# One expert's second-layer weights read and rounded in halves, and scatters moved behind GpSimd's mask in a three-layer kernel

## The reference, cut to what matters

```python
# 4 batches, 8 heads, 768 steps, 48 per head
for t in range(S):
    state = alpha[:, :, t, :, None] * state + einsum('bhd,bhe->bhde', k[:, :, t], v[:, :, t])
    y[:, :, t] = einsum('bhd,bhde->bhe', q[:, :, t], state)
x = y.transpose(0, 2, 1, 3).reshape(3072, 384)
# experts: each token goes to the expert of its largest logit
logits = (x / norm(x)) @ (emb / norm(emb)).T / tau
idx, gate = argmax(logits), softmax(logits) at idx
out[tokens of e] = gate * (maximum(x @ w1[e], 0) @ w2[e])     # w1 384x1024, w2 1024x384
# feed-forward, 384 -> 2048 -> 384
h = out @ w_in
y = where(h > 0, h, exp(minimum(h, 0)) - 1) @ w_out
```

## Time and profile before

| | us |
|---|---|
| median of 3 runs (lowest, highest) | 894.9 (894.73, 895.32) |
| the profiled execution | 891.97 |
| its span on the core | 890.3 |
| TensorE busy in it | 867.2 |
| VectorE, ScalarE, GpSimd busy | 433.6, 326.7, 284.2 |

### The profile page before, as it was taken

The page is one execution under the profiler, slowest core; times in us unless marked ns, Lnnn a source line. Parts: engine busy times, 40 slices in busy tenths (PEclk is TensorE's granted clock), DMA queues, the critical chain, the costliest instruction groups (busy, mean ns, idle before and its releaser), DMA issues. The chain is left out here.

```text
span 890.3 us, 16092 instructions
## 1 busy us (share of the span) xinstructions
PE 867.2 (97%) x5725; PEld 774.7 (87%) x5725; DVE 433.6 (49%) x810; ACT 326.7 (37%) x698; POOL 284.2 (32%) x276
## 2 busy tenths in 40 slices
PE   8999999899999999999999999999999999999996
PEld 6888887689989998998988989899989999899985
DVE  7889898752232232232226445445445445445442
ACT  4576667732223222222222323233223323233322
POOL 3235655464755574285517102002002002002001
PEclk9999999999999999999999999999999999999999
DMA  9976774778778878757517002002002002000001
GB/s 151 164 145 127 175 155 104 271 237 283 232 245 274 297 206 270 244 153 212 161 54 234 16 1 72 0 1 72 1 1 72 1 1 72 1 0 31 7 1 36
DMA packets 140575, 106.35 MB, mean 119 GB/s; under 512 B 103338, under 2 KB 129058, under 8 KB 140498
## 3 DMA queue, kind: packets, MB, share of 16 engines
q0 software_dynamic: 24896, 62.95, 22.3%
q1 hardware_dynamic: 115602, 42.37, 21.3%
HBM read 87.94 MB, written 17.35 MB: 118 GB/s over the span
## 5 line engine op out<-in xcount | busy, mean ns | idle before, releaser
L1463 POOL DMA_INDIRECT out<-of,idi x24 | 26.8, 1115 | 364.0 <-ACT of L1569 300.8
L1276 PE MATMUL bank<-WX,hdTh 128*128 (+1 forms) x496 | 128.7, 340 | 0.5 <-PEq L448 0.5
L1505 PE MATMUL bank<-xT_h,wi_h 128*128 128x512 f32 x288 | 114.1, 396 | 0.0
L1505 PE MATMUL bank<-xT_l,wi_h 128*128 128x512 f32 x288 | 113.6, 395 | 0.0
L1505 PE MATMUL bank<-xT_h,wi_l 128*128 128x512 f32 x288 | 113.3, 393 | 0.0
L1575 ACT ACTIVATE ee<-bank 128x512 f32<-128x512 f32 x96 | 57.5, 599 | 146.7 <-PE bank L1505 144.6
L1597 DVE TENSOR_SCALAR em<-ee 128x512 f32<-128x512 f32 x96 | 44.2, 460 | 136.3 <-ACT ee L1575 134.8
L1260 PE MATMUL bank<-WX,xdTh 128*128 (+1 forms) x372 | 99.7, 403 | 3.6 <-ACT xdTh L1304 2.0
L1578 ACT ACTIVATE g_h<-gg 128x512 fp32r<-128x512 f32 x96 | 60.7, 632 | 114.9 <-DVE gg L1602 113.2
L1195 POOL TENSOR_TENSOR WX<-raw_w,WX 128x3072 fp32r<-128x3072 f32 x14 | 95.6, 6830 | 15.9 <-DMA WX<-moe_w 12.6
L1606 DVE TENSOR_TENSOR g_l<-gg,g_h 128x512 fp32r<-128x512 f32 x96 | 68.5, 713 | 60.3 <-ACT g_h L1578 59.4
(11 more groups left out here) (215 smaller groups left out, 1442.0 us busy)
## 6 DMA issues: line engine op xcount, KB each, us to landing
WX<-moe_w POOLq DMA_DIRECT2D x13, 1536.0 KB, 9.8
raw_w<-moe_w POOLq DMA_DIRECT2D x13, 1536.0 KB, 7.7
xd<-sorted_x SPq DMA_DIRECT2D x31, 193.0 KB, 5.3
sorted_y<-yd SPq DMA_DIRECT2D x31, 192.5 KB, 4.1
xg<-sorted_y SPq DMA_DIRECT2D x6, 770.0 KB, 4.6
nat_a<-alpha SPq DMA_DIRECT2D x32, 144.0 KB, 4.2
nat_k<-k SPq DMA_DIRECT2D x32, 144.0 KB, 3.5
nat_q<-q SPq DMA_DIRECT2D x32, 144.0 KB, 4.5
```

Source lines behind the costliest of these rows:

```text
L1276: last = pe.matmul(y_out(t)[:, 0:DM], hdT[a][:, k * P:(k + 1) * P], WX[:, bass.ds(off + (b * WE + KD * F + k * DM), DM)], start=(k == 0 an ...
L1505: last = pe.matmul(bank[4 + i % 2][:, :], a[:, k, w], b[:, k, :], start=(k == 0 and m == 0), stop=(k == KD - 1 and m == 2))
```

## The change

It has four parts.

1. The first expert's w2 is loaded in two DMAs of 4 of its 8 blocks each (`raw_half`), with a semaphore each, instead of in one.
2. ACT rounds it in two steps of 128x1536, `Wc0` and `Wc1`. `Re0` of tile 0 and `Gq` stand between them; before, they stood behind the whole. DVE's `W3`, `W4` wait for `Wc0`, and `W5`, `W6` for `Wc1`.
3. In POOL's rounds 8 and 12, one scatter instead of three stands ahead of the mask `M1`, and the other two stand behind `Zm`. In round 14 one instead of two stands ahead of the mask, and five instead of four behind `Gm`. These three rounds are all in which the built order differs.
4. In round 14 DVE's `LA` moves from ahead of the state steps to behind `Qh1`.

```diff
@@ steps_ve
             if n == PAIRS - 2:
-                out_ = [("M0", n)] + [(x, n + 1) for x in ("G", "Kh0", "Kh1")] + [("LA", n - 1)] + sums
-                out_ += [(x, n + 1) for x in ("R", "F", "Qh0", "Qh1")] + [("Y8", PARTIAL - 1)]
+                out_ = [("M0", n)] + [(x, n + 1) for x in ("G", "Kh0", "Kh1")] + sums
+                out_ += [(x, n + 1) for x in ("R", "F", "Qh0", "Qh1")] + [("LA", n - 1), ("Y8", PARTIAL - 1)]
...
@@ steps_po
-                    out_[0:0] = [("SC", b * C + j) for j in range(2)]
-                    out_ += [("SC", b * C + j) for j in range(2, C)] + [(f"X{i}", b) for i in range(X_STEPS)]
+                    out_[0:0] = [("SC", b * C)]
+                    out_ += [("SC", b * C + j) for j in range(1, C)] + [(f"X{i}", b) for i in range(X_STEPS)]
...
                 elif b < PARTIAL - 1 and r == 4:
                     i = place_of(out_, "M1")
-                    out_[i:i] = [("SC", b * C + j) for j in range(HC, C)]
+                    out_[i:i] = [("SC", b * C + HC)]
+                    i = place_of(out_, "Zm") + 1
+                    out_[i:i] = [("SC", b * C + j) for j in range(HC + 1, C)]
...
@@ ve_a
                     if x:
-                        acA.wait(ve, "Wc", 0)
+                        acA.wait(ve, "Wc0" if i < 5 else "Wc1", n)
...
@@ ac_a
                 if kind == "Wc":
-                    ac.wait_ge(s_raw0[1], 16)
-                    return ac.activation(parts_of(0)[0][:, W12[1]], raw[1][:, :], ACT.Copy)
+                    ac.wait_ge(s_raw0[1 + i], 16)
+                    cols = slice(i * KF * DM // 2, (i + 1) * KF * DM // 2)
+                    return ac.activation(parts_of(0)[0][:, W12[1]][:, cols], raw[1][:, cols], ACT.Copy)
...
-                    if name == "Wc":
+                    if name == "Wc0":
                         d(("Re0", 0))
...
+        def raw_half(eng, e, i, done):
+
+            ks = slice(i * KF // 2, (i + 1) * KF // 2)
+            return eng.dma_start(in_three(raw[1][:, :], 1)[:, ks, :], from_dram_x(e, 1)[:, ks, :]).then_inc(done, 16)
...
@@ sp_d
-            raw_load(sp, e, 1, s_raw0)
+            for i in range(2):
+                raw_half(sp, e, i, s_raw0[1 + i])
```

More of the change, by code:

```diff
@@ L256, in build @@
         s_scat = [sem(f"s_scat{b}") for b in range(BATCHES)]
-        s_raw0 = [sem(f"s_raw0_{x}") for x in "12"]
+        s_raw0 = [sem(f"s_raw0_{x}") for x in ("1", "2a", "2b")]
         s_raw1 = [sem("s_raw1_1")]
@@ L302, in build @@
         ROUTE_PE = [({}, {"YN1": ("CT",)})] * (BATCHES - 1) + [({"YN1": ("CT",)},)]
-        ROUTE_AC = [({}, {}, {}, {"Kt1": ("Gq",)})] * (BATCHES - 2) + [({}, {}, {"Kt1": ("Gq",)}), ({"Ln0": ("SL0",), "Yn1": ("SL1",), "Ln1": ("Wc", "Gq")},)]
+        ROUTE_AC = [({}, {}, {}, {"Kt1": ("Gq",)})] * (BATCHES - 2) + [({}, {}, {"Kt1": ("Gq",)}), ({"Ln0": ("SL0",), "Yn1": ("SL1",), "Ln1": ("Wc0", "Gq", "Wc1")},)]
         ROUTE_PO = [({"Zm": ("ID",)},)] * BATCHES
```

## The result

The changed kernel takes 899.0 us (898.2 to 899.8, 6 runs) against 895.2 us (894.7 to 897.3, 6 runs) of the kernel before: a ratio of 1.0041, 95% interval 1.0031 to 1.0051. It is slower by 0.3 to 0.5%; 892.0 with a range of 890.9 to 893.9 had been forecast. Its profiled execution took 899.78 us.

What follows compares the result with a forecast made beforehand. TensorE, busy 97% of the span, was taken as the bound, so only its waits could be won. Terms 1.14 + 0 + 0 + 1.74 = 2.88 us took the median from 894.9 to 892.0, range 890.9 to 893.9.

Steps and rivals of the forecast that it cites:

- Rounds 8 and 12, 1.14 us: With the mask in time, KV to the next KT becomes 3.60 us as in round 10: 0.61 + 0.53 won.
- Rounds 9 and 13, 0 us for the moved scatters: The moved scatters land before ACT's Yn0 would be delayed (up to 102.56 in round 9), so they cost 0.
- The two rivals built on it: Moved scatters of rounds 8 and 12 held by VectorE's scan: one held, 893.6 us (0.12); both held, 896.1 us (0.06).
- the slower one: Both moved scatters held in each of two rounds, 4.1 us lost against 2.88 won: 896.1 us, chance 0.06.
- Round 14, 0 us, bounds 0 and 0.6: The third mask wait, some 0.6 us, goes, but the wait at 168.72 grows by as much: 0 won.
- the wall that is w1's load: ACT's rounding of w1 starts at 160.25 only when its load has landed, so round 14's saving stops there.
- the hold by the scan from round 8: The scatter at 92.73 took 2.20 us against 0.96 during VectorE's long scan; a moved one might be held too.
- w2 in halves, 1.74 us: The first half lands at about 169.9, so tile 0's relu wait goes: 1.74 us won, bounds 1.3 and 1.74.
- Tile 2: Rival: the relu's gain is given back at tile 2's weight load if the last scatters come no earlier: 893.5 us (0.10).
- A slower result: Whole kernel above 896.7 us, expected only in the far end of the slow case: chance 0.04.

Runs made afterwards that it cites:

- no14: Changed kernel without its part in round 14 (halves of w2, one scatter each of rounds 8 and 12 moved): 889.9 us, ratio 0.9972 to the kernel before.
- la_only: Kernel before with only LA moved behind Qh1 in round 14: 895.4 us, ratio 1.0000.
- sc14_spaced: Kernel before with one scatter of round 14 moved behind the mask, and the third behind it waiting for VectorE's scan: 892.55 us, ratio 0.9997.
- r14_w1late: Kernel before with round 14's scatter and LA moved, and w1's load issued only when Ys1 of round 14 is done: 903.1 us (one run).

## Why the prediction was wrong, by its own steps

- **Rounds 8 and 12, 1.14 us.** The mask was in time in every kernel that moves it. On a chip like the profile's the term is right: rounds 8 and 12 are 0.61 and 0.49 us shorter in no14. On the chips that timed the change it is worth nothing (1.0002): with the two scatters behind the mask `KV`'s hand-over is late (state copies 2.1 to 2.4 us behind `KV` in round 8 and 1.6 to 2.3 in round 12, against 0.91 in both in la_only). Only one profile was at hand, and it lay 2.9 us below the median of the runs. The prediction shifted its sum by that difference; it should have asked whether the waits it removes exist in the slower executions. They mostly don't in that form: in la_only `Yi1` of round 8 waits for no mask, and the loss stands between `KT` and `KV`, 7.72 us instead of 5.73:

```profile
94.56 0.94 PE L713 MATMUL bank<-mix,yts 128*128 128x128 f32 x6 [0.44 <-ACT asb L956]
...
97.05 0.79 PE L667 MATMUL bank<-vn,ktsb 128*64 128x48 f32 x20
```

- **Rounds 9 and 13, 0 us for the moved scatters.** The landing was in time; ScalarE's `Yn0` waits for no DMA there. The two rivals built on it, the slower one among them, didn't occur. But the step priced a scatter by when it lands, and not by what it does while it is issued.
- **Round 14, 0 us, bounds 0 and 0.6.** This is the step that failed. The mask wait went, 0.67 us (8.93 instead of 9.60). The five scatters behind it then cost 5.4 us in round 15 and turned the sum. The lower bound of 0 rested on the wall that is w1's load, so on the belief that nothing but the load could come later. The prediction knew of the hold by the scan from round 8 (the 2.20 us of the earlier trace rows) and took it for a danger to the landing; in round 14 the same hold was the pause that kept the row harmless. With a pause put back the term comes out as forecast: in sc14_spaced round 14 is 0.6 us shorter, and the time is that of the kernel before (0.9997).
- **w2 in halves, 1.74 us.** Mechanism and size are right. Alone it gives 1.4 us (0.5 to 2.1 by the interval), in the trace 1.77 up to the transposes of `hd`, with the half landing 2.05 us ahead of the whole where 2.1 was estimated. In the whole change it gave nothing, since the relu wait would have gone anyway with the lateness of round 15.
- **Tile 2.** Nothing was given back there: from tile 0's transposes to the end it is 713.4 us instead of 714.8.
- **The chances.** A slower result had 0.04, from a single mechanism at the landing. The case that came was in no rival. The sum of the parts that were right (no14, 2.6 us won on a chip that runs like the profile, forecast 2.88) shows that the arithmetic held there. What was missing was a term in round 14, and on the slower chips one in rounds 8 and 12 too.

Open: why TensorE's results are released late while GpSimd issues scatters without a pause, though TensorE's own rows go on at their usual pace (or whether the matmuls themselves end later than modelled); and why one chip shows none of it in rounds 8 and 12. The issuing itself is the suspect, since the DMA engines were mostly idle in r14_w1late, but no run here took issuing and travelling apart.

## What to carry to other kernels

Price a moved GpSimd scatter by its neighbours in the queue too, not by its landing alone: an unbroken row of five at their shortest period made a round 5 us longer, the same five with one pause 0.7 us. A hold that looks like waste can be the pause that something else needs; before it is removed, or moved past, try the new place with an explicit wait. And when the one profile at hand lies clearly below all timed runs, the difference is itself a finding: here some waits had another form in the runs that counted. And before a pattern of "held" and "not held" is read as a cause, look which of the two came first.

## What the runs showed of the hardware that was not expected

- In the changed kernel consumers of TensorE's results start 2 to 3 us late (ScalarE's `yts` at 161.68 and 163.22) while GpSimd issues scatters every 1.27 us; TensorE's timeline shows no gap until it needs something back. The lateness is only to be seen in the consumers' idle times and their releasers ("remote", "issue").
- A scatter that starts within VectorE's 1.76 us scan ends 0.77 us after that scan: 156.18 + 2.41 = 158.59 against 156.06 + 1.76 = 157.82. One that started ahead of it isn't held (0.96 us). By the Trainium skill, "SBUF — State Buffer", section "Who interferes with whom", a VectorE operation with two SBUF inputs leaves the write interface free that descriptor generation is inferred to need. For these scatters the rows show a hold all the same. A scatter also reads its slot numbers from SBUF, and the same section says that such an operation contends with a GpSimd instruction that reads SBUF; no run here tells which of the two accesses is held.
- After a stretch with TensorE 1.83 us busy in 5, the clock is granted at 0.50 for the next 5 us: a 3 us stand cost 5.4 us.
- Chips (or sessions) differ by 3 us for the same kernel, and not evenly: in the profiles most of it lies in rounds 8, 11 and 12 (round 8 with the old order: 9.94 us, or 10.32 to 11.66).
